# Feed-forward products placed between the steps of a recurrent scan, both chunks' levels in two PSUM banks, and attention products in 64-column tiles

## The reference

```
for t in range(768):                                   # attention: a recurrence over tokens
    y[:, :, t] = r_t . (state + outer(u * k_t, v_t))
    state      = w_t[:, None] * state + outer(k_t, v_t)
x  = y as (2, 768, 384)
xn = (x - mean) / sqrt(var + 1e-6) * g_ln              # first feed-forward layer
x  = x + relu(xn @ w_ch1) @ w_ch2                      # 384 -> 1536 -> 384
h  = relu(x @ w_in)                                    # 384 -> 1024, halves u and v
vn = (v - mean) / sqrt(var + 1e-6)
out = (u * (w_spatial @ vn + b_spatial)) @ w_out       # mixes the 768 tokens, then 512 -> 384
```

## Time and profile before

| | us |
|---|---|
| median of 3 runs | 541.44 (541.2 to 541.72) |
| the profiled execution | 542.48 |
| its span, first to last instruction | 540.7 |
| TensorE busy | 465.5 (86%) |
| its weight loads busy | 444.5 (82%) |
| VectorE, ScalarE, GpSimd busy | 214.4, 151.1, 128.7 |
| DMA queue q1 | 14.8% of 16 engines' span |

### The profile page before, as it was taken

One profiled execution on the slowest core, in us unless ns is written; L12 is line 12 of the kernel. 1 busy time (PEld: TensorE's weight loads), 2 busy tenths in 40 slices (PEclk: granted clock), 3 DMA queues, 4 the chain that ended last, 5 costly groups with the idle time before them and its releaser, 6 DMA issues.

```text
span 540.7 us, 11776 instructions
## 1 busy us (share of the span) xinstructions
PE 465.5 (86%) x4988; PEld 444.5 (82%) x4988; DVE 214.4 (40%) x492; ACT 151.1 (28%) x326; POOL 128.7 (24%) x148
## 2 busy tenths in 40 slices
PE   2587784768777787799999999999999999999997
PEld 2477673757676787689999999999999999898997
DVE  1554535164445534522145224322423267431130
ACT  3033233141233133223232123222222174311112
POOL 2445435153456345444200000000001052000000
PEclk9999999999999999999999999999999999999999
DMA  7431231212312311012000000000032010000102
GB/s 212 125 102 40 68 104 38 68 32 73 103 50 58 104 46 45 4 30 64 26 1 0 1 0 2 2 0 1 0 96 81 0 51 9 0 15 31 45 0 89
DMA packets 26553, 24.57 MB, mean 45 GB/s; under 512 B 1666, under 2 KB 23426, under 8 KB 26500
## 3 DMA queue, kind: packets, MB, share of 16 engines
q1 hardware_dynamic: 26500, 23.80, 14.8%
HBM read 21.44 MB, written 2.36 MB: 44 GB/s over the span
## 4 chain that ended last, share of the span: by engine, by line
PE 80%; DVE 8%; issue 8%; ACT 1%; POOL 1%; DMA 1%; DVEq 0%; SPq 0%; POOLq 0%; ACTq 0%
PE bank L1147 11%; PE bank L1148 10%; PE bank L1149 10%; PE low_bank L1049 8%; PE bank L1094 6%; DVE near L808 4%; PE high_bank L1149 4%; PE high_bank L1148 4%; PE high_bank L1147 4%; PE high_bank L1049 4%; PE low_bank L1147 3%; PE low_bank L1149 3%; PE low_bank L1148 3%; PE bank L1092 3%; PE low_bank L1028 2%
## 5 line engine op out<-in xcount | busy, mean ns | idle before, releaser
L1049 PE MATMUL low_bank<-rin,kin 64*64 64x32 f32 x1536 | 51.4, 291 | 48.1 <-DVE near L808 46.9
L1049 PEld LDWEIGHTS low_bank<-rin,kin 64*64 64x64 f32 x1536 | 47.2, 219 | 53.4 <-issue 50.6
L501 POOL TENSOR_TENSOR kin<-kin,wtot 128x256 f32<-128x256 f32 x60 | 52.2, 877 | 62.2 <-PE low_bank L1049 56.1
L518 POOL TENSOR_TENSOR vrstd<-vmv,half 128x1 f32<-128x1 f32 x12 | 7.7, 644 | 156.5 <-DVE vmv L979 156.5
L1094 PE MATMUL bank<-vin,score 128*128 128x48 f32 x192 | 44.6, 386 | 0.0
L1094 PEld LDWEIGHTS bank<-vin,score 128*128 128x128 f32 x192 | 44.2, 321 | 0.0
L769 DVE TENSOR_TENSOR rin<-rin,wtot 128x256 f32<-128x256 f32 x60 | 27.4, 457 | 34.7 <-PE low_bank L1049 18.7
L598 ACT COPY score<-near 64x512 f32<-64x512 f32 x24 | 14.8, 618 | 91.5 <-DVE near L808 91.3
L499 POOL TENSOR_TENSOR kin<-kin,win 128x256 f32<-128x256 f32 x12 | 12.4, 1031 | 74.7 <-PE low_bank L1049 74.7
L896 DVE SCALAR_TENSOR_TENSOR h11l<-bank,h11h 128x384 fp32r<-128x384 f32 x24 | 13.4, 558 | 38.5 <-ACT h11h L663 38.5
L511 POOL TENSOR_TENSOR ffw<-stage,ffw 128x384 fp32r<-128x384 f32 (+1 forms) x25 | 27.5, 1100 | 2.4 <-ACT ffw L584 2.4
(11 more groups left out here) (203 smaller groups left out, 1188.1 us busy)
## 6 DMA issues: line engine op xcount, KB each, us to landing
stage<-in_w SPq DMA_DIRECT2D x12, 384.0 KB, 3.3
kin<-in_kT SPq DMA_DIRECT2D x12, 256.0 KB, 4.4
rin<-in_rT SPq DMA_DIRECT2D x12, 256.0 KB, 4.3
win<-in_wT SPq DMA_DIRECT2D x12, 256.0 KB, 4.3
vin<-in_v SPq DMA_DIRECT2D x12, 192.0 KB, 3.4
out<-ob SPq DMA_DIRECT2D x12, 192.0 KB, 1.9
stage<-in_w_in SPq DMA_DIRECT2D x4, 384.0 KB, 3.2
x<-in_w_sp SPq DMA_DIRECT2D x4, 384.0 KB, 4.4
```

The source lines that it names most:

```text
L501: last = gp.tensor_tensor(k, k, wr[:, :, :, None].to_broadcast([P, NPR, m, c]), ALU.mult)
L1049: mm = te.matmul(dst[s0:s0 + Q, NPR * e + a, 0:Q // 2], kin[i % 4][lo:hi, a, s0:s0 + Q], r[:, :, 1, :], start=True, stop=True)
```

## The change

1. From round 5 on (`SLOT_F1` = slot 20), each slot of the scan also holds one `F1` and the `F2` of the step before, after the slot's levels and, in slot 3, after `attend`. That places 32 of the 48 `F1` and 31 of the 48 `F2` in the scan.
2. To free banks, from chunk 4 on the upper levels go into the other columns of `low` (`upper_bank`); the `F2` accumulators take `high` and `b_third`; in the scan `F1` has the single bank `b_first`. New waits keep TensorE out of a bank while VectorE or ScalarE read it.
3. `attend` makes each matmul as two of 64 output rows (64 columns of weights each).
4. In slot 3 `attend` comes before `turn_k`; `gain`, `turn` and `turn_k` come after the products. Transposes for the tiles run once each round from round 2, for tiles 0 to 10.
5. VectorE selects chunk `s`'s level before it multiplies chunk `s - 1`'s queries in rounds 1 to 4; `x_stats` moves to slot 0, `norm` to slot 1, `own_k` to slot 1.
6. SP's order follows the slots: `w`, `k`, `r` of chunk `s + 2` at slot 0, `v` of chunk `s + 1` at slot 1, and a weight chunk at slots given by `weight_slots`.
7. The steps of the second layer's first three groups are threaded into the 16 products left after the scan.

```diff
+ALONE = 4
-        b_f1 = [b_first, b_second]
-        b_acc = [low_bank[:, 0, :], low_bank[:, 1, :], high_bank[:, 0, :]]
-        b_vu = [high_bank[:, 1, :], b_y]
+        b_f1 = [b_first, low_bank[:, 0, :]]
+        b_acc = [high_bank[:, 0, :], high_bank[:, 1, :], b_third]
+        b_vu = [low_bank[:, 1, :], b_y]
+        def upper_bank(i, n):
+            o, c = (0 if i < ALONE else Q // 2 if n < N_MASKED else Q), min(LEVELS[n], Q)
+            return (high if i < ALONE else low)[:, :, o:o + (Q // 2 if n < N_MASKED else c)]
+        N_SLOTS = N_LOW * (NT + 1)
+        SLOT_F1 = N_LOW * (ALONE + 1)
+        N_BESIDE = N_SLOTS - SLOT_F1
+        def weight_slots(n):
+            if n < W1C // STAGE:
+                return [1 + 3 * n, 2 + 3 * n]
+            m = n - W1C // STAGE
+            return [SLOT_F1 - 1 + 2 * m, SLOT_F1 + 2 * m]
...
# SP
-            for i in range(2, NT):
-                load_w(i)
-                load_k(i)
-                load_r(i)
-                load_chunk(i - 1)
-                load_v(i - 1)
+            for k, s, j in slots_of_scan():
+                if j == 0 and 4 <= s + 2 < NT:
+                    load_w(s + 2)
+                    load_k(s + 2)
+                    load_r(s + 2)
+                if j == 1 and 3 <= s + 1 < NT:
+                    load_v(s + 1)
+                for n, part in weight_parts(k):
+                    if part == 1:
+                        load_chunk(n + 2)
...
# TensorE, near_level and attend
+                    if n == 1:
+                        te.wait_ge(own_placed, i + 1)
+                    if i > ALONE and n <= N_MIDDLE:
+                        te.wait_ge(middle_placed, N_MIDDLE * (i - 1) + n)
+                    elif i > ALONE:
+                        te.wait_ge(blocks_placed, i)
...
-                        te.matmul(b_y[:, at:at + 2 * HD], rin[i % 4][:, a, :], wide[:, a, :], start=True, stop=False)
+                        for lo, hi in HALF:
+                            te.matmul(b_y[lo:hi, at:at + 2 * HD], rin[i % 4][:, a, lo:hi], wide[:, a, :],
+                                      start=True, stop=False)
                     for e in range(2):
-                        mm = te.matmul(b_y[:, at + e * HD:at + (e + 1) * HD], score[:, NPR * e + a, :],
-                                       vin[i % 3][:, 2 * a + e, :], start=first(i), stop=first(i) or e == 1)
+                        for lo, hi in HALF:
+                            mm = te.matmul(b_y[lo:hi, at + e * HD:at + (e + 1) * HD], score[:, NPR * e + a, lo:hi],
+                                           vin[i % 3][:, 2 * a + e, :], start=first(i), stop=first(i) or e == 1)
...
# TensorE, the order of a slot
+                if j == 3 and s >= 1:
+                    attend(s - 1)
+                n = f1_of(k)
+                if n is not None:
+                    first_product(n // NF, n % NF)
+                    if n:
+                        second_product((n - 1) // NF, (n - 1) % NF)
+                if j == 0 and s >= 2 and carries(s - 2):
+                    gain(s - 2)
+                if j == 2 and s >= 2:
+                    turn(s - 2, "XT", (s - 2) // TG, (s - 2) % TG)
+                if j == 3 and s >= 1 and carries(s - 1):
+                    turn_k(s - 1)
...
# VectorE: waits before the selects, and the slot's end
+                if i > ALONE:
+                    level_done(dve, i - 1, N_LOW)
...
+                n = f1_of(k)
+                if n is not None:
+                    h1_lo(n)
+                    if n and n % NF == 0:
+                        add_f2(n // NF - 1)
```

More of the change, by code:

```diff
@@ L525, in _ @@
             gp.memset(half[:, :], -0.5)
[L526 to L536, removed]
+            for k, s, j in slots_of_scan():
+                if s < NT:
+                    k_left(s, j)
+                if s >= 1 and j < N_HIGH:
+                    k_left(s - 1, N_LOW + j)
+                if s >= 2 and j == 1:
+                    inv_std(mv, rstd, s - 2, x_var_ready, x_rstd_ready)
+                for n, part in weight_parts(k):
+                    weight_lo(n, part)
             inv_std(mv, rstd, NT - 1, x_var_ready, x_rstd_ready)
@@ L662, in h1_hi @@
                     act.wait_ge(f2_done, n - 1)
-                sc.activation(h1[n % 2][0][:, :], b_f1[n % 2][:, 0:GT], ACT.Relu).then_inc(h1_hi_ready, 1)
-            for n in range(EARLY):
-                h1_hi(n)
+                sc.activation(h1[n % 2][0][:, :], f1_bank(n)[:, 0:GT], ACT.Relu).then_inc(h1_hi_ready, 1)
+            own_k(0)
+            for k, s, j in slots_of_scan():
+                if j == 0 and s >= 2:
+                    if carries(s - 2):
+                        take_kt(s - 2)
+                    take_x(s - 2)
+                if j == 1 and s + 1 < NT:
+                    own_k(s + 1)
+                if j == 2 and s >= 1:
+                    place_near(s - 1)
+                    place_blocks(s - 1, 6)
+                    if s >= 2 and carries(s - 2):
+                        widen(s - 2)
+                if j == 3 and s >= 2:
+                    turned_hi(s - 2, "XT", (s - 2) // TG, (s - 2) % TG)
+                for n, part in weight_parts(k):
+                    weight_hi(n, part)
+                if f1_of(k) is not None:
+                    h1_hi(f1_of(k))
             take_x(NT - 1)
-            tr, vu = TG, 0
+            tr, vu = NT - 1, 0
             for step, g, a in STEPS:
@@ L915, in decay_plan @@
                 return []
-            decays(0, 0)
[L918 to L937, removed]
-                        next_state(s - 2)
[L939 to L943, removed]
@@ L944, in _, with add_f2 @@
-            for n in range(EARLY):
-                h1_lo(n)
+            def add_f2(g):
+                dve.wait_ge(f2_done, NF * (g + 1))
+                for tt in range(TG):
+                    i = TG * g + tt
+                    ve.tensor_tensor(x[:, i, :], b_acc[tt][:, 0:D], x[:, i, :], ALU.add).then_inc(x2_ready, 1)
+            decays(0, 0)
+            for k, s, j in slots_of_scan():
+                if s < NT:
+                    r_right(s, j)
+                if s > ALONE and j < N_HIGH:
+                    r_right(s - 1, N_LOW + j)
+                if j == 0 and s < NT:
+                    own_select(s)
+                if s < NT:
+                    select(s, j)
+                if 1 <= s <= ALONE and j < N_HIGH:
+                    r_right(s - 1, N_LOW + j)
+                if j < N_MIDDLE and s >= 1:
+                    select(s - 1, N_LOW + j)
+                for i, n in decay_plan(s, j):
+                    decays(i, n)
+                if j == 0 and s >= 2:
+                    for part in range(3):
+                        x_stats(s - 2, part)
+                    if carries(s - 2) and not first(s - 2):
+                        decay_state(s - 2)
+                if j == 1 and s >= 2:
+                    if carries(s - 2):
+                        next_state(s - 2)
+                    norm(s - 2)
+                if j == 3 and s >= 2:
+                    turned_lo(s - 2, "XT", (s - 2) // TG, (s - 2) % TG)
+                n = f1_of(k)
[3 more added lines that the diff above has]
+                        add_f2(n // NF - 1)
@@ L957, in _ @@
                     tr += 1
[L958 to L960 removed]
                 elif step == "F1":
                     n = NF * g + a
[L963 to L966, removed]
+                    h1_lo(n)
+                    if n == N_BESIDE:
+                        norm(NT - 1)
+                    elif n - N_BESIDE - 1 < 4:
+                        bias_split(n - N_BESIDE - 1)
                 elif step == "X2":
[L968 to L971, removed]
+                    add_f2(g)
                 elif step == "V":
```

215 lines of the change are left out of this document (98 added, 117 removed).

## The result

The changed kernel takes 455.56 us (median of 4 runs, 453.97 to 456.80), the one before 541.58 (541.20 to 542.05): a ratio of 0.841, 95% interval 0.838 to 0.844. The profiled execution took 455.75, with a span of 454.0. I had forecast 475, in a range of 452 to 506, so the result lies 3.6 us above the lower end.

A forecast was written before the change was run, and what follows sets the result against it. The scan was taken as a chain with gaps at 1.2 GHz, TensorE filling the rest. 92.1 us up to round 5, 189 for rounds 5 to 12 and 193.3 after sum to 474.4, 475 for the median; range 452 to 506.

The forecast's parts named there:

- rival 1: In the scan, the clock falls between products: 500 us if once a round, 528 if every second slot; chance 0.15.
- rival 2: The clock never rises in the scan: 581 us, slower than before; chance 0.04, including cases as good as it.
- Rival 3: In the scan, other engines set the slots, the single `F1` bank or select waits adding 1 us each: 507 us; chance 0.05.
- Rival 4: The halves of `attend` don't overlap, costing 15 us: 490 us; its chance lies within the 0.68 for 458 to 490.
- my sum, 458 to 490: Whole kernel: the forecast's own case, summed to 474.4 us of span, 475 for the median; chance 0.68.
- rival 5: Form changes cheap at 2.4 GHz and levels a little faster: 455 to 460 us; chance 0.08 for better than 458.
- +3.7 for the wait: Round 2: +4.2 us for `turned_lo` and `turn_k` after `w` arrives, -0.5 for the `v` transfer.
- the 2.7 us that I left for `w(7)` in slot 19: Round 4: waiting left after `decays` and `turned_lo`, as `w(7)` lands some 2 us into `attend`.
- `own_term` 0.81 and six near levels 5.1: Rounds 5 to 12: these small matmuls keep today's price in us per round; halved they would be 3.0 less.
- changes of form: Rounds 5 to 12: ten tile-form changes a round with gaps of 0.2 us, 2.0 us a round.
- the first slot at 1.2 GHz: Start of rounds 5 to 12: 3 us added for the first slot or two at the low clock.
- About 1 us to spare: Each scan slot: one `F1` and one `F2`, 3.15 us, cover the wait for both selects with this reserve.

The follow-up runs named there:

- e8: The kernel before, nothing moved, with six wide products whose result nobody reads added to each slot from round 5 on: 523.12 us, ratio 0.967.
- e13: The kernel before with 64-column `attend` tiles, `w` loaded further ahead and six thrown products in each slot from round 5 on: 491.44 us, ratio 0.908.
- e3: The changed kernel with the scan's `F1` and `F2` both reduced to one of three passes: 428.68 us, ratio 0.793.
- e3b: The changed kernel with only `F2` reduced to one of three passes in the scan: 438.35 us, ratio 0.810.
- e1: The kernel before with only `attend` changed, to 64-column tiles: 518.08 us, ratio 0.957.
- e4: The changed kernel with `w` loaded one chunk further ahead: 442.86 us, ratio 0.819.
- e10: The changed kernel with `weight_hi` counted for each half of a chunk, and GpSimd's wait on it: 447.86 us, ratio 0.827.
- e2: The changed kernel with `attend` back in 128-column tiles: 470.07 us, ratio 0.869.
- e5: The changed kernel with group 0's second and third `X2T` step one product later, apart from tile 11's transpose: 452.36 us, ratio 0.835.

## Why the prediction came out as it did

**The mechanism was right.** The products fill TensorE's waits, they hold the clock at 2.4 GHz through rounds 5 to 12, and the small matmuls profit. `e8` shows the clock's share without the placing, `e13` what all the rest brings without it. Rivals 1 and 2 did not occur in the scan; `e3` and `e3b` show that rival 1 comes in this order when products are taken out. Of rival 3 there is a little: TensorE waits 6.2 us in all from 90 to 230 us. Rival 4 fell with `e1`.

**The size was not.** 455.6 lies outside "my sum, 458 to 490", to which I gave 0.68, and inside rival 5, "better than the sum", 455 to 460, which had 0.08. The forecast held by the width of its range; the chances were badly placed.

**Up to round 5: 88.9 for 92.1.** Round 2 was 22.1 us for 18.7 before (I had +3.7 for the wait and about -0.9 for the selects), round 3 18.4 for 22.1, so 3.7 less where my terms give about 5, and round 1 14.0 for 17.2, 3.2 less for about 2. Round 4 became 15.5 us for 27.3, 11.8 less where my terms give about 9: the 2.7 us that I left for `w(7)` in slot 19 did not come. So errors of 1 to 3 us both ways lie in the 3.2 us. `e4` and `e10` price what stayed: of their 12.7 and 7.7 us, 9.5 and 3.8 lie before round 5. The cause behind the second I had not seen: the change splits a chunk's halves over two slots while the low part still waits for both high ones.

**Rounds 5 to 12: 166.5 for 189.** This is the term that was mis-sized: "`own_term` 0.81 and six near levels 5.1: I leave both at today's price, since columns don't matter to them". From equal prices for 32 and 64 columns I concluded that the clock doesn't matter either. It does: a four of records every 58 ns for 107, so a round's levels and diagonal term (56 fours) cost 3.3 us for 5.9. That is 2.7 a round, some 19 us over the scan. I had named this bound ("halved they would be 3.0 less") and taken the wrong end of it. The changes of form were too dear as well: across each of the ten in a round of the changed kernel the starts are 0.15 to 0.27 us apart, about 0.1 more than like records would be, so by estimate 1 us a round for my 2.0. A steady round took 21.2 us on average (105.8 us for rounds 6 to 10) for my 23.9, and the first slot at 1.2 GHz (3 us) didn't come either: the clock had risen at 88.1 us behind the narrow `attend`. In `e2`, with the wide one, it was low there, and round 5 took 24.6 us for 22.3, of which 1.0 is the wide `attend` itself. Levels 19, changes of form 8 and first slot 3 make some 30 us for the 22.5 measured; against them stand the 6.2 us of waits, and about 1 us that I did not trace.

Here the Trainium skill ("TensorE: Matmul & The Clock Gate", Part 1) has a floor of about 25 ns between starts for small matmuls; the trace after has 17 a record on average, and 0.39 us for 12 records of `attend`, 33 ns each with 48 and 96 columns. The measurement decides: for float32 records in 64x64 tiles, of which four start 6 to 7 ns apart, there is no floor at 25. The 25 to 27 of the earlier trace rows looked like this floor and were a quarter of the 107 ns from four to four at 1.2 GHz.

**The slot's reserve.** "About 1 us to spare" was too much, by `e3b` about 0.5; with all products in place the waits that got through are the 6.2 us above.

**After the scan: 198.5 for 193.3.** 3.6 us are the wait of the neighbours `XT` and `X2T` and the fall of the clock behind it (`e5`: 3.2). The wait was made by the new order; that the clock fell behind it was chance as far as these runs tell. I had moved the steps without asking which of them share the transpose bank. The other 1.6 us I did not trace.

## What to carry to other kernels

Read TensorE's pace from the starts of like matmuls before believing the clock column, and ask of each stretch at 1.2 GHz whether wide products could stand in it: the gain is then not only the time of what is moved, but the faster small work around it. When steps are threaded in by hand, check every queue for a wait that now covers two slots (a half that waits for the whole, two users of one bank side by side, a load behind a chunk): three such waits were worth 19 us here, some of it clock. Where a row leaves a price between two bounds, ask which resource makes it; that it doesn't depend on the columns doesn't say that it doesn't depend on the clock.

## What the runs showed of the hardware that I had not expected

- The granted clock in the profile is 1.00 until its first entry, whatever the engine really does: over rounds 5 to 12 of the kernel before it says 1.00 while the fours of level records go 107 ns apart, and behind them products 0.32 us apart; in `e4` it says 1.00 at 34 us, where a level takes 0.85 us.
- 64x64 tiles of float32 with 32 columns: four records start 6 to 7 ns apart, and a new four comes every 58 ns at 2.4 GHz and every 107 ns at 1.2. A level of 32 records is 0.47 and 0.85 us.
- Two matmuls of 64 weight columns are together 1.7 times as fast as one of 128 when the moving side has 48 or 96 columns: a quarter of `attend` 1.28 and 0.75 us at 1.2 GHz, 0.67 and 0.39 at 2.4.
- Behind those narrower attends the clock rose eleven times for 3 to 7 us (`e1`); with the wide ones it did not rise once in the scan of the kernel before, and once before round 5, for 3.4 us, in `e2`.
- A wait of 1.97 us behind dense products was followed by 3.4 us at 1.2 GHz in the changed kernel; the same wait in `e3`, `e4` and `e10` was not.
